# Routing and scattering tokens per tile inside the delta rule, with late zeroing of the rows behind each expert's count

## The reference

```python
for t in range(S):                                   # delta rule
    y[:, :, t] = einsum('bhd,bhde->bhe', q[:, :, t], state)
    v_old = einsum('bhde,bhd->bhe', state, kt)
    state = state + bt * einsum('bhd,bhe->bhde', kt, vt - v_old)
x = y.transpose(0, 2, 1, 3).reshape(3072, 384)       # tokens

e_idx = argmax(x @ w_gate, axis=1)                   # one of 8 experts
gate_w = softmax(x @ w_gate)[e_idx]
eom = sigmoid(x @ w_output_gate)
for e in range(8):
    out[mask] = gate_w * eom[mask, e] * (maximum(x[mask] @ w1[e], 0) @ w2[e])

h = maximum(maximum(x @ W1, x @ W2), x @ W3)         # last layer
return h @ w_out
```

## Time and profile before

| | us |
|---|---|
| median of 3 runs | 1154.94 (1149.84 to 1159.45) |
| the profiled execution | 1154.56 |
| its span | 1152.8 |
| PE busy in the span | 1012.1 (88%) |
| delta rule, until the last copy of logits ends | about 494 |
| from there to the first transposition of the experts | about 56 |
| mean granted TensorE clock | 0.963 of full |

### The profile page before, as it was taken

The page is one execution under the profiler, slowest core; times in us unless marked ns, Lnnn a source line. Parts: engine busy times, 40 slices in busy tenths (PEclk is TensorE's granted clock), DMA queues, the critical chain, the costliest instruction groups (busy, mean ns, idle before and its releaser), DMA issues. The chain is left out here.

```text
span 1152.8 us, 30762 instructions
## 1 busy us (share of the span) xinstructions
PE 1012.1 (88%) x13236; PEld 887.3 (77%) x13236; DVE 482.1 (42%) x922; ACT 366.7 (32%) x731; POOL 324.4 (28%) x226
## 2 busy tenths in 40 slices
PE   1789999999998999810899999999599999999999
PEld 1678878888887888710799999999578888888888
DVE  3455555555555554360344344344242314242321
ACT  0255545555554555410222222222121212122211
POOL 2232333233422421046545255453420101000000
PEclk9999999999999999955899999999889999999999
DMA  8712121220212100016324344432211000100000
GB/s 267 269 54 63 28 60 40 62 63 26 63 40 62 41 20 19 2 42 232 136 81 155 122 151 151 150 124 82 89 49 35 28 34 20 34 20 28 10 19 28
DMA packets 59394, 86.37 MB, mean 75 GB/s; under 512 B 29200, under 2 KB 54288, under 8 KB 56720
## 3 DMA queue, kind: packets, MB, share of 16 engines
q1 hardware_dynamic: 53616, 48.46, 13.1%
q0 software_dynamic: 5664, 36.18, 9.2%
HBM read 61.82 MB, written 22.81 MB: 73 GB/s over the span
## 5 line engine op out<-in xcount | busy, mean ns | idle before, releaser
L1029 PE MATMUL hb<-early,last_h 128*128 128x512 f32 x648 | 203.8, 396 | 4.7 <-ACT o_sb L1143 3.5
L1029 PEld LDWEIGHTS hb<-early,last_h 128*128 128x128 f32 x648 | 120.5, 189 | 30.8 <-ACT o_sb L1143 2.7
L1029 PE MATMUL hb<-early,last_l 128*128 128x512 f32 x324 | 126.9, 392 | 0.0
L480 DVE TENSOR_TENSOR p<-bank,cf 128x512 f16<-128x512 f32 x96 | 66.0, 688 | 45.1 <-PE bank L283 44.8
L283 PEld LDWEIGHTS bank<-t,n_hi 64*64 64x64 f16 x2688 | 66.2, 111 | 21.1 <-issue 5.7
L1167 DVE TENSOR_TENSOR m<-hb,m 128x512 f32<-128x512 f32 x36 | 24.9, 691 | 131.4 <-PE hb L1029 131.4
L283 PE MATMUL bank<-t,n_hi 64*64 64x64 f16 x2688 | 71.6, 195 | 4.6 <-issue 3.9
L1029 PE MATMUL ob<-wo_h,early 128*128 128x384 f32 x288 | 74.2, 335 | 0.0
L1029 PEld LDWEIGHTS hb<-early,last_l 128*128 128x128 f32 x324 | 61.3, 189 | 13.2
L951 POOL TENSOR_TENSOR late<-w_raw,late 128x3072 fp32r<-128x3072 f32 x8 | 54.4, 6801 | 56.3 <-DVE late L923 56.0
L585 POOL COPY x_all<-y_tile 128x384 f32<-128x384 f32 x24 | 12.1, 503 | 205.3 <-ACT y_tile L451 205.3
(11 more groups left out here) (155 smaller groups left out, 2191.4 us busy)
## 6 DMA issues: line engine op xcount, KB each, us to landing
w_raw<-w POOLq DMA_DIRECT2D x14, 1536.0 KB, 7.6
kq_t<-qh SPq DMA_DIRECT2D x24, 256.0 KB, 3.3
x_sorted<-zeros SPq DMA_DIRECT2D x32, 192.0 KB, 1.9
x_in<-x_sorted SPq DMA_DIRECT2D x29, 192.0 KB, 2.4
y_sorted<-y_sb SPq DMA_DIRECT2D x28, 192.0 KB, 1.9
k_raw<-kt_in SPq DMA_DIRECT2D x24, 192.0 KB, 3.5
k_own<-kh SPq DMA_DIRECT2D x24, 192.0 KB, 3.3
v_in<-vh SPq DMA_DIRECT2D x24, 192.0 KB, 3.3
```

Of the source, the lines that this page charges most:

```text
L480: dve.tensor_tensor(p16[st][:], pb, mask_of(lv), ALU.mult).then_inc(prod_out[st], 1)
L1029: ins = pe.matmul(out, a[x], b[y], start=first and i == 0, stop=last and i == 2, skip_group_check=True)
```

## The change

`route_and_sort` is gone. Each expert has a fixed area of `AREA` = 26 tiles in a larger `xs`, so a token's row is the expert's area start plus the number of tokens of that expert before it. This needs only a running count (`counted`), so each tile is routed and scattered while the delta rule runs:

- At `lg` DVE copies the logits and then finds the expert in four small instructions (`best`, `score`, `top`, `chosen`). A new piece `rank` on PE (CHAIN slot 15) multiplies `chosen` and `counted` with constant matrices, a new piece `slot` on DVE (slot 16) turns that into the row numbers `rows_at` and adds to `counted`, and a new piece `send` on POOL (slot 17) scatters `y_tile`, which is now doubled. POOL's copy to `x_all` is gone. The next step's first `ks` on PE now waits for the first instruction of `slot`, since both use the same PSUM bank.
- The router's product has 16 instead of 128 columns.
- The first expert's weights are split in 6 pieces of 512 columns in steps 2 to 7 (NORM parts 10, 11, 12 at slots 4, 12 and 14), and POOL loads the second expert's weights in step 10.
- SP no longer zeroes `xs` early. It writes 14 zero tiles to the tail of `ys`, spread over steps 2 to 11. Behind the delta rule it reads expert 0's count and zeroes the 2 x 128 rows behind it; in `experts` it zeroes those of expert e + 1 while expert e runs.
- Behind the walk PE adds up the totals and DVE makes the table in ten instructions. The gates are computed by DVE and ACT at the start of `experts`. SP loads two or three numbers of the table at each expert, and stores three unused tiles of `ys` first (LEAD = 3).

The diff, cut to its core:

```diff
-    CHAIN = {0: ("ks", 0), 2: ("z", 0), 4: ("up", 0), 6: ("ks", 1), 8: ("z", 1), 10: ("up", 1), 12: ("yt", 0), 14: ("lg", 0)}
-    NORM = {1: [0], 2: [1], 3: [2], 5: [3], 6: [4], 7: [5], 8: [6], 9: [7, 8], 10: [9]}
+    CHAIN = {0: ("ks", 0), 2: ("z", 0), 4: ("up", 0), 6: ("ks", 1), 8: ("z", 1), 10: ("up", 1), 12: ("yt", 0), 14: ("lg", 0),
+             15: ("rank", 0), 16: ("slot", 0), 17: ("send", 0)}
+    NORM = {1: [0], 2: [1], 3: [2], 4: [10], 5: [3], 6: [4], 7: [5], 8: [6], 9: [7, 8], 10: [9], 12: [11], 13: [13], 14: [12]}
...
-        with sp.Fori(0, MAXB + 1) as g:
-            sp.dma_start(xs[bass.ds(P * g, P), :], zeros[:]).then_inc(xs_zeroed, 16)
-
-        with sp.Fori(TILES, MAXB + 1) as g:
-            sp.dma_start(ys[bass.ds(P * g, P), :], zeros[:]).then_inc(xs_zeroed, 16)
...
+            for i in range(BLANK * (k - 2) // (STEPS - 2), BLANK * (k - 1) // (STEPS - 2)):
+                at = P * (LEAD + TILES + i)
+                sp.dma_start(ys[at:at + P, :], zeros[:]).then_inc(zeroed, 16)
+        sp.wait_ge(zeroed, 16 * BLANK)
+        sp.wait_ge(tabled, 8)
+        row = sp.value_load(table[0:1, 2, 0:1], min_val=0, max_val=N)
+        sp.dma_start(xs[bass.ds(row, MINB * P), :].rearrange("(n p) x -> p n x", p=P),
+                     zeros[:].unsqueeze(1).broadcast_to((P, MINB, X))).then_inc(zeroed, 16)
+        sp.wait_ge(zeroed, 16 * BLANK + 16)
...
-                    pe.wait_ge(logit_out[st], k)
+                    pe.wait_ge(routed[st], 5 * k - 1)
...
+            elif what == "rank":
+                pe.wait_ge(chosen_ready[st], k + 1)
+                if 2 * k + st >= 1:
+                    pe.wait_ge(counted_ready, 2 * k + st)
+                pe.sem_inc(passed_pe, 1)
+                pe.matmul(out[:, X + P - E:X + P], tri16, chosen[:, 2 * k + st, :], start=True, stop=False, skip_group_check=True)
+                pe.matmul(out[:, X + P - E:X + P], ones16, counted[:], start=False, stop=True,
+                          skip_group_check=True).then_inc(rank_done[st], 1)
...
+                dve.tensor_reduce(best[:, st:st + 1], logits[:, to, 0:E], AX.X, ALU.max).then_inc(routed[st], 1)
+                dve.wait_ge(routed[st], 5 * k + 1)
+                dve.scalar_tensor_tensor(out=score[st][:], in0=logits[:, to, 0:E], scalar=best[:, st:st + 1],
+                                         in1=cf[:, CF_IOTA:CF_IOTA + E], op0=ALU.is_equal, op1=ALU.mult).then_inc(routed[st], 1)
+                dve.wait_ge(routed[st], 5 * k + 2)
+                dve.tensor_reduce(top[:, st:st + 1], score[st][:], AX.X, ALU.max).then_inc(routed[st], 1)
+                dve.wait_ge(routed[st], 5 * k + 3)
+                dve.tensor_scalar(chosen[:, to, :], score[st][:], top[:, st:st + 1], None, ALU.is_equal).then_inc(chosen_ready[st], 1)
+            elif what == "slot":
+                to = 2 * k + st
+                dve.wait_ge(rank_done[st], k + 1)
+                dve.tensor_tensor(place[st][:], yb[st][:, X + P - E:X + P], chosen[:, to, :], ALU.mult).then_inc(routed[st], 1)
...
-            if what == "yt":
-                pool.wait_ge(y_out[st], 2 * k + 2)
-                pool.tensor_copy(x_all[:, 2 * k + st, :], y_tile[st][:]).then_inc(x_out[st], 1)
+            if what == "send":
+                to = 2 * k + st
+                pool.wait_ge(slot_ready[st], k + 1)
+                if k >= 1:
+                    pool.wait_ge(rows_sent[st], 16 * k)
+                pool.indirect_dma_start(xs, bass.IndirectOffsetOnAxis(ap=rows_at[:, to:to + 1], axis=0),
+                                        y_tile[par][st][:], None).then_inc(rows_sent[st], 16)
...
+            if e + 1 < E:
+                row = sp.value_load(table[0:1, 2, e + 1:e + 2], min_val=P * AREA * (e + 1), max_val=P * AREA * (e + 1) + N)
+                sp.dma_start(xs[bass.ds(row, MINB * P), :].rearrange("(n p) x -> p n x", p=P),
+                             zeros[:].unsqueeze(1).broadcast_to((P, MINB, X))).then_inc(zeroed, 16)
+            off = sp.value_load(table[0:1, 0, e:e + 1], min_val=0, max_val=AREA * e)
+            end = sp.value_load(table[0:1, 1, e:e + 1], min_val=MINB * (e + 1), max_val=MAXB)
```

More of the change, by code:

```diff
@@ L31 @@
 F2 = 768
[L32 removed]
+MINB = 2
+MAXB = TILES + (E - 1) * MINB
 EPS = 1e-6
@@ L132, in attention_and_router @@
     z = single("z", [P, NP, 2, D], F32)
-    y_tile = single("y_tile", [P, X], F32)
+    y_tile = double("y_tile", [P, X], F32)
     y_t = single("y_t", [P, KX, P], F32)
-    zeros = sb("zeros", [P, X], F32)
+    best = sb("best", [P, 2], F32)
+    score = single("score", [P, E], F32)
+    top = sb("top", [P, 2], F32)
+    place = single("place", [P, E], F32)
+    rows_at = sb("rows_at", [P, TILES], U32)
+    counted = sb("counted", [P, E], F16)
+    more = sb("more", [P, E, TILES], F32)
+    blocks = sb("blocks", [P, E], F32)
+    sums = sb("sums", [P, E, E], F32)
+    ends = sb("ends", [P, E], F32)
+    begins = sb("begins", [P, E], F32)
+    logits, chosen, slot_f, shift, table, zeros, zeroed = routing
     bank = [[ctx.enter_context(nc.psum_tensor(f"bank{st}{i}", [P, 512], F32)) for i in range(3)] for st in range(2)]
@@ L746, in experts @@
-def experts(nc, ctx, sems, cf, table, xs, ys, weights, w1, w2, w_in, w_out):
+        for st in range(2):
+            pool.wait_ge(rows_sent[st], 16 * STEPS)
+def experts(nc, ctx, sems, cf, routing, gate, slots, xs, ys, weights, w1, w2, w_in, w_out):
     def sem(name):
@@ L768, in experts @@
     y_sb = sb("y_sb", [P, X])
+    logits, chosen, slot_f, shift, table, zeros, zeroed = routing
+    lg, og = logits[:, :, 0:E], logits[:, :, E:2 * E]
+    best_of = sb("best_of", [P, TILES])
+    spread = sb("spread", [P, TILES, E])
+    exps = sb("exps", [P, TILES, E])
+    picked = sb("picked", [P, TILES, E])
+    denom = sb("denom", [P, TILES])
+    z_gate = sb("z_gate", [P, TILES])
+    exp_gate = sb("exp_gate", [P, TILES])
+    product = sb("product", [P, TILES])
+    moved = sb("moved", [P, E])
     h_bank = [ctx.enter_context(nc.psum_tensor(f"h_bank{i}", [P, 512], F32)) for i in range(2)]
@@ new lines, in build @@
+        weights.early = [sb(f"early{i}", [P, KX * F], F32R) for i in range(4)]
+        routing = (sb("logits", [P, TILES, 2 * E]), sb("chosen", [P, TILES, E], F16), sb("slot_f", [P, TILES]), sb("shift", [P, E]),
+                   sb("table", [P, 3, E], I32), sb("zeros", [P, X]), ctx.enter_context(nc.semaphore("zeroed")))
+        xs = nc.dram_tensor("x_sorted", (P * (E * AREA + MAXB), X), F32, kind="Internal").ap()
+        ys = nc.dram_tensor("y_sorted", (P * (LEAD + MAXB), X), F32, kind="Internal").ap()
@@ L1255, in build @@
+        with ExitStack() as part:
+            ch = part.enter_context(nc.sbuf_tensor("ch", [P, CH_END], F16))
+            wr = part.enter_context(nc.sbuf_tensor("wr", [P, KX, 2 * E], F32))
+            attention_and_router(nc, part, ctx, kt_in, kh, qh, vh, bh, cf_in, ch_in, wr_in, cf, ch, wr, routing, xs, ys, weights, w1, w2)
         weights.last = [[sb(f"last{i}_{h}", [P, KX * F2], F32R)[:] for h in "hl"] for i in range(3)]
         with ExitStack() as part:
-            experts(nc, part, ctx, cf, table, xs, ys, weights, w1, w2, w_in, w_out)
+            experts(nc, part, ctx, cf, routing, gate, slots, xs, ys, weights, w1, w2, w_in, w_out)
```

329 lines of the change are left out of this document (156 added, 173 removed).

## The result

The changed kernel takes 1208.8 us (median of 4 runs, 1202.1 to 1215.2) where the kernel before takes 1157.2 beside it: ratio 1.045, 95% interval 1.035 to 1.054. It is slower, outside the range, and on the side that I gave 2 chances in 100. The profiled execution took 1213.75 us, its span is 1212.1.

What follows compares the result with a forecast made beforehand. Outside its gaps the kernel was taken to run at PE's pace, the gap bound by DVE's routing, then POOL's issues. 1154.56 - 45.1 (gap) + 7.5 (delta rule) = 1117 us, range 1106 to 1130.

Steps and rivals of the forecast that it cites:

- the side that I gave 2 chances in 100: Whole kernel: the outcome that the change makes it slower, chance 0.02.
- The gap, -45.1: Between last logits copy and first `x_in` load: load issued at 502.3 instead of 547.44, 45.1 us less (42 to 46.5).
- the estimate of 0.07 beside the sum: DVE's 8-element instructions: 0.07 us each by the skill's figures, end chain about 1 us shorter; the sum used 0.17.
- SP's branch: Behind the last logits: totals, table, count and zero write, then the barrier, end last, at 502.3, after POOL's scatter.
- The delta rule, +7.5: Delta rule with routing inside: 4 + 2 + 2 - 0.5 = 7.5 us longer, between 0 and 20.
- POOL is idle just while DVE routes: Delta rule: POOL's scatter waits for row numbers ahead of `kn` and `beta_mask`; argued against the DVE and POOL collision.
- The clock: Delta rule: PE's clock falling below 1.00 was listed as a sign of error, with no size given.
- DVE's part: Delta rule: small routing instructions mostly fit DVE's idle time; with `rank`, 0.2 to 0.4 a step, about 4 us over 12.
- weights pieces: Delta rule: splitting the first expert's weights on DVE in six steps costs six times 0.3, 2 us.
- DVE against POOL: Rival, chance 0.13: DVE and POOL block each other in the delta rule; 1146 us at worst, about 1130 if half.
- What comes behind the first load stays as it is: Experts and last layer, after the first `x_in` load: same time as now, difference 0.
- SP's extra work costs nothing: Experts' loop: SP's extra number loads and zero writes fall where SP waits, costing nothing; 24 us if late by 3 each.

Runs made afterwards that it cites:

- e1: The changed kernel with POOL's scatter of a tile one slot later in the walk (18 for 17), behind `n_kb_a`: 1137.5 us, ratio to before 0.981.
- e2: The changed kernel with SP's loads of `kq_t` and `v_in` issued ahead of `k_own`, POOL's order unchanged: 1139.1 us, ratio to before 0.986.
- f1: The changed kernel with both the scatter at slot 18 and SP's loads of q and v ahead of `k_own`: 1140.0 us, ratio to before 0.984.
- h0: g3 run once more without a further change, as the base for h1 and h2: 1132.6 us, ratio to before 0.979.
- b0: The kernel before, unchanged, profiled once more on the same chip as the runs beside it: 1159.4 us.
- f4: f1 with the first expert's weights split after the table and the second expert's loaded after the walk, both outside the delta rule: 1154.2 us, ratio 0.997.
- g1: f1 with every SBUF tile of the stages behind the delta rule at its address in the kernel before: 1130.3 us, ratio to before 0.979.
- f3: f1 with one unused tile of 32 bytes a partition allocated behind the routing tiles: 1140.5 us, ratio to before 0.986.
- g2: f1 with SP's zero writes behind its last delta-rule load and the second expert's weights loaded one step later: 1142.5 us, ratio to before 0.989.
- g3: The changes of g1 and g2 together, on f1: 1130.7 us, ratio to before 0.980.
- h1: g3 with all 24 scatters issued behind the walk, routing left in the delta rule: 1172.6 us; sends wrong rows, so read in the delta rule only.
- g4: The kernel before with only a second load of the first expert's weights (2 x 1.5 MB) added at index 8: 1156.6 us, ratio 1.000.
- h2: g3 with routing computed behind the walk and scatters to fixed rows at their old place: 1123.9 us; read in the delta rule only.

## Why the prediction was wrong, point by point

- **The gap, -45.1: right** (-45.0), in its size and its chain. The small DVE instructions take 0.15 to 0.23 us (the estimate of 0.07 beside the sum is not seen), rows and table are ready at 1.8 and 4.5 us after the copy (forecast 2.0 and 4.8), and SP's branch ends last.
- **The delta rule, +7.5: wrong, +94.3.** The step that failed is the cost of the wait that the change puts on POOL. I wrote "POOL is idle just while DVE routes" and "it has 85 of 120 us idle", and took idle time for free time. An engine's queue is in order: the scatter's wait holds what is behind it, `n_kb_a`, for which SP's `k_own` waits, behind which SP's loads of q and v stand, for which PE waits. I traced what waits for the row numbers, and never who waits for what is queued behind the waiting instruction. The slack to ask for was in the trace before: 3 us, against a wait of 7.73. The chain is worth 71 to 75 us of the 94 (e1, e2, f1).
- **The clock** was named as a sign of error ("if the clock in the delta rule falls below 1.00") but had no price. At 0.87 over 400 us, 52 us of full clock are missing, but part of that lies in PE's idles, where it costs nothing. By the trace's clock records some 38 us of it fall where PE is busy (an estimate: half of PE's busy time at 0.50), about four tenths of the 94; the nine idles themselves are 51. The Trainium skill, TensorE: Matmul & The Clock Gate (Terms), prices throttled time as its length times the missing share of the clock; the trace agrees, the 32 products of `gram` take 3.68 us at 0.50 and 1.96 at 1.00.
- **DVE's part: about right in size, not in its places.** Six of e1's later steps are 36.1 to 36.9 us with all of the routing in, and 4 us was the forecast for twelve. The second to fourth step cost 2 to 3 us each (h0 against b0), which it did not have; weights pieces nothing that shows (forecast 2). In all 6 to 10 for the routing where 7.5 stood. That the two agree is in part luck. The delta rule of the mended kernels still ends 14 to 24 us behind the profiles of before, and 9 to 13 of that have no term in the sum.
- **DVE against POOL**: the split's pieces on DVE take 0.68 us alone and up to 1.81 beside POOL (e1, after), as the earlier trace rows let expect, but f4, without the pieces, has no shorter delta rule. The rival's 13 to 29 us did not come.
- **"What comes behind the first load stays as it is": wrong by 9.9**, of which 9.7 are the tiles' addresses (f1 against g1). I compared instructions and counts, which are the same, and not where their operands lie.
- **"SP's extra work costs nothing": right**; the experts' stage has no new wait.
- With the mends the forecast's gain from the gap is kept: the best version, g1, takes 1130.3 us, 2.1% (1.7 to 2.5) under the kernel before, where the changed one is 4.5% over it; that is 13 us above the forecast.

## What to carry to other kernels

For each wait that a change adds, go down the queue behind the waiting instruction until something other engines wait for, go on through their queues (a DMA queue is one of them), and compare the wait's length with the slack of that last one in the trace of before; idle time of the engine says nothing. Put a late wait behind everything that frees a buffer: here one slot made 71 us. And a change that allocates tiles ahead of others moves these others: compare a stage that was not touched, by mean duration of one instruction, before looking for its cause in the work.

## What the runs showed of the hardware

- The same product of 128x512 takes 396 or 404 ns by where its operands lie in SBUF (g1 and after), all starts being multiples of 32 bytes (worked out from the tiles' sizes). The Trainium skill, SBUF — State Buffer (Specifications (TRN2), the row on cachelines), has lines of 16 bytes, by which there would be no difference; the measurement decides. 32 bytes moved by f3 gave 401.
- At a burst of 3 MB over 9 us PE stops for 3.1 to 4.3 us (e2, e1, f3, g1, g2, g3, h0, h1; 2.2 to 2.5 in f1, g4 and h2), with nothing in the semaphores to see. Why is argued, not shown.
- An idle of PE of 4 to 6 us is followed by 5 to 9 us at 0.50 (after, e2), so that it costs one and a half to two times its length.
